# Scores of chunks 5 to 23 as one f32r product per head, with the terms of split q and k stacked along the contraction

## The reference

```python
for t in range(S):
    m_new = np.maximum(f_gate[:, :, t] + m, i_gate[:, :, t])
    f_stab = np.exp(f_gate[:, :, t] + m - m_new)
    i_stab = np.exp(i_gate[:, :, t] - m_new)
    C = f_stab[:, :, None, None] * C + i_stab[:, :, None, None] * np.einsum('bhd,bhe->bhde', vt, kt)
    n = f_stab[:, :, None] * n + i_stab[:, :, None] * kt
    h_tilde = np.einsum('bhde,bhe->bhd', C, qt)
    denom = np.maximum(np.abs(np.einsum('bhd,bhd->bh', n, qt)[:, :, None]), 1.0)
    y[:, :, t] = 1.0 / (1.0 + np.exp(-o_gate[:, :, t])) * h_tilde / denom
```

## Time and profile before

| | |
|---|---|
| median of three runs | 752.84 us (752.45 to 753.73) |
| profiled execution, its time | 752.84 us |
| its span | 751.1 us |
| PE busy | 742.5 us (99%) |
| DVE, ACT, POOL busy | 463.4, 306.9, 185.1 us |
| granted TensorE clock | 0.998 of full speed |

### The profile page before, as it was taken

How to read it: one execution, slowest core, us unless ns; L and a number is a source line. 1 busy time by engine, 2 the same in 40 slices (tenths; PEclk the granted TensorE clock), 3 DMA queues, 4 the chain that set the end, 5 groups by cost and what they waited for, 6 DMA issues and landing times.

```text
span 751.1 us, 11653 instructions
## 1 busy us (share of the span) xinstructions
PE 742.5 (99%) x4472; PEld 656.8 (87%) x4472; DVE 463.4 (62%) x792; ACT 306.9 (41%) x646; POOL 185.1 (25%) x213
## 2 busy tenths in 40 slices
PE   9899999999999999999999999999999999999998
PEld 6899999999988888888888888888888888888886
DVE  7887887799787858875887547634342423324232
ACT  5675644644564446444643447321212112121211
POOL 6697154164343324332442000000000000000000
PEclk9999999999999999999999999999999999999999
DMA  9972311422222203220200180030201002010100
GB/s 243 293 197 103 121 66 66 125 69 91 94 93 81 98 32 117 75 96 22 95 1 1 55 263 1 0 120 1 78 0 62 17 1 77 1 36 0 36 1 35
DMA packets 30407, 55.66 MB, mean 74 GB/s; under 512 B 3176, under 2 KB 19024, under 8 KB 29968
## 3 DMA queue, kind: packets, MB, share of 16 engines
q1 hardware_dynamic: 29888, 54.49, 23.4%
q10 hardware_dynamic: 464, 0.43, 0.2%
HBM read 46.96 MB, written 7.95 MB: 73 GB/s over the span
## 4 chain that ended last, share of the span: by engine, by line
PE 92%; DVE 3%; POOL 2%; ACT 1%; issue 1%; DMA 1%; SPq 0%; DVEq 0%; ACTq 0%; POOLq 0%
PE bank L767 26%; PE bank L730 22%; PE bank L745 6%; PE bank L653 6%; PE bank L747 5%; PE bank L746 5%; PE bank L782 3%; PE bank L784 3%; PE bank L783 3%; PE bank L749 3%; PE bank L750 3%; PE bank L661 2%; PE bank L669 2%; PE bank L691 1%; PE bank L703 1%
## 5 line engine op out<-in xcount | busy, mean ns | idle before, releaser
L730 PE MATMUL bank<-x_split,w_hi 128*128 128x512 f32 (+2 forms) x560 | 167.7, 367 | 1.9 <-ACT x_split L871 1.9
L730 PE MATMUL bank<-x_split,w_lo 128*128 128x512 f32 (+2 forms) x336 | 120.4, 360 | 0.0
L913 ACT ACTIVATE g_full<-bank 128x512 f32<-128x512 f32 (+2 forms) x112 | 59.8, 534 | 139.9 <-PE bank L730 138.9
L730 PEld LDWEIGHTS bank<-x_split,w_hi 128*128 128x128 f32 x560 | 102.8, 189 | 14.1 <-ACT x_split L871 2.1
L1151 DVE SCALAR_TENSOR_TENSOR g_full<-g_full,beta,bank 128x512 f32<-128x512 f32 (+2 forms) x112 | 74.7, 667 | 40.1 <-ACT g_full L913 39.6
L1132 DVE TENSOR_TENSOR g_lo<-g_full,g_hi 128x512 fp32r<-128x512 f32 (+2 forms) x112 | 77.5, 692 | 29.5 <-ACT g_hi L922 28.8
L1172 DVE TENSOR_TENSOR best<-bank,first_of_max 128x512 f32<-128x512 f32 x36 | 24.9, 691 | 102.5 <-PE bank L767 76.1
L745 PE MATMUL bank<-g_hi,wproj 128*128 128x512 f32 (+2 forms) x224 | 83.9, 374 | 0.8 <-DVE g_lo L1132 0.8
L922 ACT ACTIVATE g_hi<-g_full 128x512 fp32r<-128x512 f32 (+2 forms) x112 | 63.1, 563 | 47.9 <-DVE g_full L1151 47.7
L747 PE MATMUL bank<-g_hi,wproj 128*128 128x512 f32 (+2 forms) x224 | 80.5, 359 | 0.0
L746 PE MATMUL bank<-g_lo,wproj 128*128 128x512 f32 (+2 forms) x224 | 80.3, 359 | 0.0
(11 more groups left out here) (135 smaller groups left out, 1445.2 us busy)
## 6 DMA issues: line engine op xcount, KB each, us to landing
u_bcast<-u_scratch SPq DMA_DIRECT2D x21, 512.0 KB, 3.9
kv<-in_kv SPq DMA_DIRECT2D x24, 324.0 KB, 3.0
q_t<-in_q_t SPq DMA_DIRECT2D x24, 180.0 KB
k_t<-in_k_t SPq DMA_DIRECT2D x72, 60.0 KB
out<-final SPq DMA_DIRECT2D x5, 640.0 KB, 3.8
wproj_raw<-in_w_out SPq DMA_DIRECT2D x4, 640.0 KB, 9.2
o_gate<-in_o_gate SPq DMA_DIRECT2D x4, 640.0 KB, 4.8
w_raw<-in_w_max SPq DMA_DIRECT2D x2, 1152.0 KB, 6.4
```

What stands on the lines that cost most here:

```text
L730: ins = pe.matmul(ps[:, 0:cols], w[:, a, f], xs[:, x, 0:cols], start=(m == 0), stop=(m == 7))
L913: act.activation(gf[:, n % GF_SLOTS, 0:cols], hid[j % HID_BANKS][:, 0:cols], ACT.Relu, scale=-1.0).then_inc(neg_done, 1)
```

## The change

From chunk 5 on (`STACK = UNSPLIT`), q and k are each split by ACT and DVE in a high and a low f32r part (`parts`: q low, q high, k high, k low, 120 partitions x 384 each). SP then copies them inside SBUF: for each head, the 40 rows of three terms come to lie on 120 partitions, in `qks[:, 0]` for q (high, high, low) and in `qks[:, 1]` for k (high, low, high). So one f32r product over 120 partitions gives q_high.k_high + q_high.k_low + q_low.k_high. The copy takes nine DMAs (`TERMS` x `KH`), each of 40 partitions x 2 x 384 elements, 120 KB. There is one `qks`, so the copies for a chunk wait until the scores of the chunk before are done.

q and k now have two buffers; both are loaded by `load_qk(ch)`, which waits for the carry of chunk ch - 2, and k comes in one DMA from chunk 5 on. In SP's list, `load_kv` and `load_u` of a chunk come first, then the copies for the chunk before it, then `load_qk`; `store_rows(b)` and `load_o` move one chunk ahead. The split of chunk ch is made in the last group of chunk ch - 2. The three old k buffers of chunks 0 to 4 share SBUF with the new tiles.

```diff
+STACK = UNSPLIT
+TERMS = 3
...
-            pack * [("pack", ch + 1, 1)]]
+            pack * [("pack", ch + 1, 1)] + (STACK <= ch + 2 < NCH) * [("stack", ch + 2)]]
...
+        def load_qk(eng, ch):
+
+            c = ch % 2
+            wait(eng, scored, NG * (ch - 1) if ch < STACK else 0)
+            wait(eng, carry_out, ch - 2)
+            eng.dma_start(qk[0:KR, c, 0, :], q_t[ch]).then_inc(qk_loaded[c], 16)
...
+            else:
+                eng.dma_start(qk[0:KR, c, 1, :], k_t[ch].rearrange("a d t -> (a d) t")).then_inc(qk_loaded[c], 16)
...
+        def stack(eng, ch):
+
+            eng.wait_ge(scored, NG * ch)
+            eng.wait_ge(qk_split, ch - STACK + 1)
+            for n in range(TERMS):
+                pair = (slice(1, 3), slice(1, 4, 2), slice(0, 3, 2))[n]
+                for a in range(KH):
+                    eng.dma_start(qks[n * D:(n + 1) * D, :, a * NK:(a + 1) * NK, :].rearrange("p n g t -> p n (g t)").bitcast(F32),
+                                  parts[a * D:(a + 1) * D, pair, :].bitcast(F32)).then_inc(stacked, 16)
...
             for ch in range(SLOTS + 1, NCH):
-                load_chunk(sp, ch)
+                load_kv(sp, ch)
                 load_u(sp, ch)
+                if ch > STACK:
+                    stack(sp, ch - 1)
+                load_qk(sp, ch)
                 if ch == FIRST[1] + SLOTS - 1:
                     load_o(sp, 2)
                 for b in range(NBLK - 2):
-                    if ch == min(FIRST[b + 2] + SLOTS, NCH) - 1:
+                    if ch == FIRST[b + 2] + 1:
                         store_rows(b)
...
+                    if ch < STACK:
+                        pe.wait_ge(qk_loaded[ch % 2], qk_loads(ch))
+                    else:
+                        pe.wait_ge(stacked, 16 * TERMS * KH * (ch - STACK + 1))
...
+                            if ch < STACK:
+                                lhs, rhs = kt[ch % SLOTS][0:KR, at, :], qk[0:KR, ch % 2, 0, of * L:(of + 1) * L]
+                            else:
+                                lhs, rhs = qks[0:KR, 1, at, :], qks[0:KR, 0, at, :]
+                            ins = pe.matmul(ps[:, k * L:(k + 1) * L], lhs, rhs, start=True, stop=True)
...
+                if kind == "stack":
+                    act.wait_ge(qk_loaded[ch % 2], qk_loads(ch))
+                    act.wait_ge(scored, NG * SLOTS)
+                    wait(act, stacked, 16 * TERMS * KH * (ch - STACK))
+                    act.activation(parts[0:KR, 1:3, :], qk[0:KR, ch % 2, :, :], ACT.Copy).then_inc(qk_high, 1)
...
+                if kind == "stack":
+                    dve.wait_ge(qk_high, ch - STACK + 1)
+                    dve.tensor_tensor(parts[0:KR, 0:4:3, :], qk[0:KR, ch % 2, :, :], parts[0:KR, 1:3, :].bitcast(F32),
+                                      ALU.subtract).then_inc(qk_split, 1)
```

More of the change, by code:

```diff
@@ L67 @@
 RING_BANKS = 3
-QK_LOADS = 16 * (1 + KH)
 CREDIT2 = 2
@@ L158, with qk_loads @@
 W2_LOW_AT = {5: (0,), 6: (1, 2), 7: (3, 4), 8: (5, 6), 9: (7, 8), 10: (9, 10), 11: (11,)}
+def qk_loads(ch):
+    return sum(16 * (1 + KH) if n < STACK else 32 for n in range(ch % 2, ch + 1, 2))
 class Links:
@@ L212, in build @@
         att_at = cursor[0]
-        qt, _ = sb("q_t", [128, SLOTS, NK, L], F32)
-        kt, _ = sb("k_t", [128, SLOTS, KH * NK, L], F32)
+        qk, _ = sb("qk_t", [128, 2, 2, NK * L], F32)
+        qks, qks_at = sb("qk_stacked", [128, 2, KH * NK, L], F32R)
+        parts, parts_at = sb("qk_parts", [128, 4, NK * L], F32R)
         ub, _ = sb("u_bcast", [128, SLOTS, H, L], F32)
@@ L235, in build @@
         end_at = cursor[0]
+        kt = [sb(f"k_t{c}", [128, KH * NK, L], F32, at)[0]
+              for c, at in enumerate((qks_at, qks_at + KH * NK * L * 4, parts_at))]
         pick, _ = sb("pick_head", [128, H, L], F32, prob_r_at)
@@ L323, in build @@
         w_split = sem("weights_split")
-        qk_loaded = [sem(f"qk_loaded{c}") for c in range(SLOTS)]
+        qk_loaded = [sem("qk_loaded_a"), sem("qk_loaded_b")]
+        qk_high = sem("qk_high")
+        qk_split = sem("qk_split")
+        stacked = sem("stacked")
         u_loaded = [sem(f"u_loaded{c}") for c in range(SLOTS)]
@@ L476, in _ @@
             sp.wait_ge(k_cleared[0], 1)
-            load_chunk(sp, 0)
+            load_qk(sp, 0)
+            load_kv(sp, 0)
             sp.wait_ge(k_cleared[1], 1)
-            load_chunk(sp, 1)
+            load_qk(sp, 1)
+            load_kv(sp, 1)
             load_w1(sp, 0, range(3))
@@ L483, in _ @@
             sp.wait_ge(k_cleared[2], 1)
-            load_chunk(sp, 2)
+            load_qk(sp, 2)
+            load_kv(sp, 2)
             load_o(sp, 1)
@@ L491, in _ @@
             load_w1(sp, 2, range(3))
-            load_chunk(sp, 3)
+            load_qk(sp, 3)
+            load_kv(sp, 3)
             sp.wait_ge(u_stored[0], 16)
@@ L508, in _ @@
                             load_o(sp, b + 3)
+            stack(sp, NCH - 1)
             sp.wait_ge(x_ready, NCH)
@@ L651, in attention @@
                         for k in range(HG):
-                            h = g * HG + k
-                            ins = pe.matmul(ps[:, k * L:(k + 1) * L], kt[0:KR, c, h % KH * NK + h // KH, :], qt[0:KR, c, h // KH, :],
-                                            start=True, stop=True)
+                            of, n = divmod(g * HG + k, KH)
+                            at = n * NK + of
+                            if ch < STACK:
+                                lhs, rhs = kt[ch % SLOTS][0:KR, at, :], qk[0:KR, ch % 2, 0, of * L:(of + 1) * L]
+                            else:
+                                lhs, rhs = qks[0:KR, 1, at, :], qks[0:KR, 0, at, :]
+                            ins = pe.matmul(ps[:, k * L:(k + 1) * L], lhs, rhs, start=True, stop=True)
                         ins.then_inc(scored, 1)
@@ L1358 @@
         "i_gate": i_gate.reshape(B * H, S),
-        "q_t": nine(q).transpose(0, 2, 3, 1, 4).reshape(NCH, KR, NK, L),
-        "k_t": nine(k).transpose(0, 2, 3, 1, 4),
+        "q_t": nine(q).transpose(0, 2, 3, 1, 4).reshape(NCH, KR, NK * L),
+        "k_t": nine(k).transpose(0, 2, 3, 1, 4).reshape(NCH, KH, D, NK * L),
         "kv": np.concatenate([tokens(k), tokens(np.concatenate([v, np.ones_like(v[..., :1])], axis=3))], axis=2),
```

17 lines of the change are left out of this document (8 added, 9 removed).

## The result

| | before | after |
|---|---|---|
| median | 752.64 us | 772.94 us (771.3 to 774.38, four runs) |
| profiled span | 751.1 us | 772.4 us |
| mean granted TensorE clock | 0.998 | 0.987 |

The changed kernel takes 1.0261 times as long (95% interval 1.0245 to 1.0277). The forecast was 741.2 us, faster, with 734 to 748 as the range; it is wrong in sign.

A forecast was written before the change was run, and what follows sets the result against it. PE was taken to bound the attention, with DVE a near second in block 2 alone. Span 751.1 - 17.0 + 1.4 + 0.8 + 3.0 + 0.2 = 739.5 us, plus 1.74 for the execution: 741.2 us, range 734 to 748.

The forecast's parts named there:

- The price of the scores: PE, chunks 5 to 23: a head takes 112 ns instead of 224, gaining 17.0 us over 152 heads.
- A: PE's scores: an f32r product of 128 columns costs the same 224 ns as f32; 756.5 us, slower; chance 0.13.
- C: PE's scores: loads overlap neighbouring products better, a head costs 76 ns; 5.5 us less, 736 us; chance 0.08.
- The place of the first long wait: Chunk 9's scores: copies 2.2 us late behind store_rows(1); 3.0 us lost, with ACT's hold at chunk 10's copy.
- the wait at the end of block 0: PE's wait for DVE's g_lo grows from 0.49 to near 2 us; 1.4 us lost.
- ACT's 0.84 us: ACT's added copy of 120 x 768 per split chunk takes about 0.84 us.
- DVE's 951 ns: Trace time of the same subtraction where POOL rests, placed in layer 2; 1.05 us taken for each split.
- the time from a block's store to the landing of the copies behind it: SP's queue after block 1: 3.11 MB at 269 GB/s take 11.6 us from 140.0, then 0.8 to land.
- the three later boundaries: After blocks 2 to 4 the next scores come later behind the store; 0.2 us lost together.
- Rival D: Copies inside SBUF over 40 partitions run at half rate, over 8 us a chunk; 760 us or more; chance 0.05.
- rival B: DVE's in-order waits for ACT's copy hold the relay in block 2 and at boundaries; 747 us; chance 0.12.
- 0.8 us on block 2: Loss in block 2, where DVE's work rises to 59.0 us beside PE's 59.3; between nothing and about 3.

The follow-up runs named there:

- stores back: The changed kernel with store_rows and load_o moved back to where they stood before, behind the next chunk's loads and copies; all else as changed: 753.87 us, 1.0012 of before.
- the last experiment: Old store order, DVE's subtraction moved to the front of the next chunk's scores: 751.21 us from chunk 5 on, 748.8 us from chunk 14 on.
- subtraction alone: The changed kernel without copies, f32r scores of high parts only, ACT's copy left out from chunk 7 on, DVE's subtraction kept: 750.35 us, 0.9952 of before.
- ACT's copy alone: The changed kernel without copies, f32r scores of high parts only, DVE's subtraction left out from chunk 7 on, ACT's copy kept: 744.34 us, 0.988 of before.

## Why the prediction was wrong

**Right.** The price of the scores: 0.84 us a chunk where 0.9 was forecast, and 0.9 gained per chunk where nothing else was added. Rivals A and C are refuted by the same rows. The place of the first long wait, chunk 9 behind `store_rows(1)`, and the wait at the end of block 0, 1.71 us where about 2 was named, were also right. ACT's 0.84 us was exact. (DVE's 951 ns are from 454 to 470 us, at the end of layer 1 and not in layer 2; POOL rests there too.)

**The step that failed first: the time from a block's store to the landing of the copies behind it.** The sum had 13.0 us for it (139.36 to 152.4). By it chunk 9 would be some 2 us late, and the three later boundaries, where PE comes to the scores 13.6 to 14.1 us behind the store, would hardly wait; they had 0.2 us together. It took 15.8, 17.6, 17.4 and 15.4 us, and PE waited 4.5 us at chunk 9 and 9.1 at the others, with 25 us in which ACT stood at its copy.

Two parts of the working were wrong. "Three DMAs of that kind take SP 1.08 us to issue, nine 3.2": they were not of that kind. Those read HBM, the copies read SBUF, and one takes 0.81 us instead of 0.36. But this alone doesn't make the 15.8 us, since the last copy was issued at 152.8, 9.3 us behind the store. From there the chain shows 6.5 us until the landing:

```profile
152.81 6.49 DMA qk_stacked<-qk_parts
```

and the table of stretches of the kernel after has, for these microseconds,

```profile
146.00:150.00 4.00, 3.86 (x43) 3.59 (x42) 3.96 (x8) 3.97 (x5) 1.78 (x2) 1.00 0.96 317
...
156.00:159.30 3.30, 0.00 (x0) 0.00 (x0) 0.00 (x0) 0.00 (x0) 2.30 (x4) 1.00 1.09 199
```

The second part is the amount and the rate: 3.11 MB at 269 GB/s were forecast, and 3.8 MB moved in the 15.8 us, at 239 GB/s. The sum counted only what stands ahead of the copies' end in SP's list; q, k, `kv` and `u_bcast` of the next chunk were issued from 153.6 us on, and some 0.7 MB of them moved beside the last copies. How the 2.8 us divide between the two parts isn't shown.

Rival D had the outcome in part, waits of 2 to 5 us and a time of over 760 us, but at one chunk of each block and by another mechanism. Its half rate is not what the runs show: where nothing but copies is under way, as here in the kernel with the stores back, the DMA engines are busy for less than half of the time, at SP's pace of 120 KB in 0.81 us.

```profile
242.00:247.00 5.00, 4.73 (x42) 3.80 (x41) 4.96 (x9) 1.24 (x4) 1.82 (x2) 1.00 0.46 153
```

**What was not in the sum: the clock.** Four of these waits were followed by stretches at the lower clock, 8.5 us in all. The sum took every wait at its own length. The bound on the losses should have said that a wait of PE of some microseconds may cost up to as much again: the wait of 1.77 us at chunk 21 was followed by 3.4 us at half clock, 1.7 us lost.

**The split on DVE and ACT, rival B.** This step failed apart from the first and would have sufficed: with the stores back no copy is waited for, and 753.87 us still lies outside of the range. The forecast put 0.8 us on block 2 and nothing on blocks 1, 3, 4 and 5, "while the relay has slack". Without any copy the two steps took 10.7 us from chunk 5 on (-14.8 against -4.1), 4.9 of it in block 2 and 1.5, 2.2 and 1.3 in the later stretches. Busy shares hid this. DVE is idle for 17 of 76 us there, but DVE takes its list in order, and for one split its list gets 0.93 us of waiting for ACT, 1.54 of work and a longer `g_lo` behind it, 3 us in one piece, a step ahead of `prob` and `carried`. For these PE waits; in the kernel with the stores back, its table of waits has

```profile
PE bank L715 <- DVE prob L1107: 4.9, 5, 2.1
```

while in blocks 3 to 5 hardly a wait for `g_lo` is left: the relay of layer 1 had the slack that the forecast gave it, the path from scores to values had not. Rival B had the place, DVE's waits for ACT's copy, and about half the price, though it looked for it in the relay. In block 2 even PE's own gain came to only 1.6 of 3.6 us, for PE then waits for DVE's `carried` and POOL's `prob`. The forecast had argued with DVE's sum of 59.0 us there, and drew from it "between nothing and about 3"; it was 6.9 (+3.3 where -3.6 was PE's part), or 9.1 with the copies and the half clock at 156.5 us.

**The account.** From chunk 5 to layer 2, in the table's numbers: PE's gain -17.1 (19 x 0.9); PE's waits for DVE and POOL before any split +2.3, 2.0 of it in block 2, which leaves -14.8; ACT's copy +0.9; DVE's subtraction +5.4; the two in one place +4.4; the copies, in SP's old order, +2.2, of which 1.7 are the half clock behind a wait for `prob`; in all -1.9. SP's changed order adds 20.0, the sum of the five differences between after (+18.1) and the kernel with the stores back (-1.9). In those 20.0, 14.2 us are waits of PE for the copies and about 6.8 the additional time at half clock (17.1 less 3.4 us, halved); these two add up to slightly more, perhaps because a part of the wait takes up delays which the other kernel shows elsewhere. Block 0's end adds 1.2 to 2.3 us (1.71 - 0.49, and 1.04).

**Open.** What the 4.4 us are made of that the two steps cost together: the last experiment removed DVE's waits for ACT and the longer subtraction beside POOL, and apart from the clock the time hardly changed. Why a copy inside SBUF takes SP twice as long: the runs show only that it does, at two sizes. Why full DMA engines moved 199 GB/s at 156 us and 317 at 146. Copies issued by another engine's queue weren't tried.

## What to carry to other kernels

A time for a DMA is taken from a DMA between the same memories; where the profile has none, the bound above is a multiple, and one queue's issues are summed against the time of a chunk before anything is put in front of them. What the queue issues behind a transfer counts too, as long as it moves beside it. A step added to an engine that is 77% busy isn't free by its average: what counts is the piece in a row (its wait for the engine before it, its own time beside its neighbours, what stands behind it) against the slack at that one place. And work that PE gives up is gained only where PE is alone at the bound: applied from chunk 14 on, the same change gives 0.6%, from chunk 5 on, with the best order found, 0.2%.

## What the runs showed of the hardware

- A DMA from SBUF to SBUF of 40 partitions keeps SP for 0.74 us with 60 KB and 0.81 with 120 KB; one of 40 x 384 from HBM 0.36. Copies of 120 KB alone, at that pace, keep the DMA engines busy for 46% at 153 GB/s.
- An f32r product of 120 x 128 with its weight load goes at 105 ns (8 in 0.84 us, full clock).
- After a wait of 1.8 to 4.5 us, PE ran for 3.4 us or twice that at the lower clock. In other kernels a wait of 2.1 us was followed by one such stretch (stores back), waits of 2.2 us by one (subtraction alone) or by none (ACT's copy alone).
- The same DVE subtraction takes 0.95 us beside POOL's `state_decayed`. Where it starts together with `v_weighted`, either it takes 1.54 us and `v_weighted` 0.73, or it takes 0.96 and `v_weighted` 1.56. In the kernel with the subtraction alone, where it began beside POOL's select on `u_bcast`, it took 1.84. So a few nanoseconds in the start, or a move by one step, went with a change of 0.6 to 0.9 us.
